# Attention on one core: q and k split as one 128-row tile, their copies made in two rounds, and heads stored in pairs

## The reference

```python
scores = q @ k.T / sqrt(64)                     # q, k, v: (4, 8, 576, 64) float32
thresh = scores.max(-1) - tau
attn = exp(where(scores >= thresh, scores, -1e9) - scores.max(-1))
attn = attn / (attn.sum(-1) + 1e-9)
x = (attn @ v) -> rows (4 * 576, 8 * 64)        # then the two expert layers
```

## Time and profile before

| what | value |
|---|---|
| median of three runs | 1363.23 us (1362.61 to 1364.46) |
| the profiled execution, its own time | 1361.96 us |
| its span, first to last instruction | 1359.8 us |
| attention | from 0 to about 385 us of the span |
| one iteration of the loop (four heads) | about 45 us |
| q1 queue (SP), share of 16 DMA engines' span | 20.2% |
| DMA share between 205 and 250 us | 0.41, 97 GB/s |

### The profile page before, as it was taken

One profiled execution on the slowest core, in us unless ns is written; L12 is line 12 of the kernel. 1 busy time (PEld: TensorE's weight loads), 2 busy tenths in 40 slices (PEclk: granted clock), 3 DMA queues, 4 the chain that ended last, 5 costly groups with the idle time before them and its releaser, 6 DMA issues.

```text
span 1359.8 us, 22119 instructions
## 1 busy us (share of the span) xinstructions
PE 1276.0 (94%) x7777; PEld 1147.4 (84%) x7777; DVE 652.3 (48%) x1256; ACT 560.0 (41%) x987; POOL 521.3 (38%) x372
## 2 busy tenths in 40 slices
PE   5999999999984799999999999994999999999998
PEld 4999999999842789989999998993999899899897
DVE  7999999999815211212121121114455445545443
ACT  3888888888842232333323333331221112112111
POOL 1777777777831252443434334344341101000000
PEclk9999999999987799999999999996999999999999
DMA  5443434343330332423324233233221102000000
GB/s 119 90 97 96 99 94 100 89 105 89 95 97 0 101 126 92 155 100 119 125 103 143 90 128 129 103 117 124 72 83 55 47 1 70 16 0 23 15 1 24
DMA packets 117483, 113.31 MB, mean 83 GB/s; under 512 B 74736, under 2 KB 84528, under 8 KB 117424
## 3 DMA queue, kind: packets, MB, share of 16 engines
q1 hardware_dynamic: 103552, 77.37, 20.2%
q0 software_dynamic: 6080, 19.93, 4.5%
q10 hardware_dynamic: 7792, 15.21, 3.1%
HBM read 81.90 MB, written 19.92 MB: 75 GB/s over the span
## 4 chain that ended last, share of the span: by engine, by line
PE 80%; DVE 8%; issue 4%; ACT 2%; POOL 2%; DMA 1%; SPq 1%; DVEq 0%; POOLq 0%; ACTq 0%
PE h_ps L629 31%; PE y_ps L647 10%; PE y_ps L646 10%; PE y_ps L648 10%; PE o_acc L516 4%; PE ring L477 3%; PE ring L490 3%; PE ring L478 2%; PE ring L491 2%; DVE k_parts L907 2%; PE t_ps L607 2%; ACT probs L711 1%; DVE neg_max L877 1%; PE logits_t_ps L558 1%; DVE q_lo L905 1%
## 5 line engine op out<-in xcount | busy, mean ns | idle before, releaser
L629 PE MATMUL h_ps<-x_hi,region_a 128*128 128x384 f32 (+1 forms) x1408 | 341.9, 315 | 2.8 <-DVE x_lo L1021 2.8
L1115 POOL TENSOR_TENSOR probs_lo<-probs,probs_hi 128x576 fp32r<-128x576 f32 x160 | 226.2, 1422 | 89.3 <-ACT probs_hi L719 89.1
L629 PEld LDWEIGHTS h_ps<-x_hi,region_a 128*128 128x128 f32 x1408 | 246.0, 189 | 9.2 <-DVE x_lo L1021 3.6
L629 PE MATMUL h_ps<-x_lo,region_a 128*128 128x384 f32 (+1 forms) x704 | 220.3, 313 | 0.0
L1031 DVE SCALAR_TENSOR_TENSOR h_lo<-h_ps,h_hi 128x256 fp32r<-128x256 f32 (+1 forms) x128 | 62.8, 491 | 318.7 <-ACT h_hi L805 318.7
L808 ACT ACTIVATE h_hi<-act_out 128x384 fp32r<-128x384 f32 (+1 forms) x112 | 53.7, 479 | 316.0 <-DVE act_out L1040 316.0
L647 PE MATMUL y_ps<-region_b,h_hi 128*128 128x512 f32 x448 | 176.3, 393 | 0.0
L648 PE MATMUL y_ps<-region_b,h_lo 128*128 128x512 f32 x448 | 176.0, 393 | 0.0
L646 PE MATMUL y_ps<-region_b,h_hi 128*128 128x512 f32 x448 | 175.7, 392 | 0.0
L1101 POOL TENSOR_TENSOR region_b<-stage,region_b 128x1024 fp32r<-128x1024 f32 x40 | 95.7, 2394 | 172.4 <-ACT region_b L700 172.3
L805 ACT ACTIVATE h_hi<-h_ps 128x256 fp32r<-128x256 f32 (+1 forms) x128 | 56.0, 438 | 243.4 <-PE h_ps L629 238.7
(11 more groups left out here) (161 smaller groups left out, 2438.8 us busy)
## 6 DMA issues: line engine op xcount, KB each, us to landing
stage<-in_moe_w SPq DMA_DIRECT2D x56, 512.0 KB, 3.5
expert_rows<-rows_out ACTq DMA_DIRECT2D x8, 768.0 KB, 3.8
q_hi<-q_hi SPq DMA_DIRECT2D x32, 160.0 KB
k_ones<-k_parts SPq DMA_DIRECT2D x32, 160.0 KB
qk_nat<-in_q SPq DMA_DIRECT2D x32, 128.0 KB, 2.7
qk_nat<-in_k SPq DMA_DIRECT2D x32, 128.0 KB, 2.7
v_nat<-in_v SPq DMA_DIRECT2D x16, 256.0 KB, 2.9
early<-in_moe_w SPq DMA_DIRECT2D x16, 256.0 KB, 3.1
```

Of the source, the lines that this page charges most:

```text
L629: mm = pe.matmul(h_ps[:, c % 2, 0:width], wt, x[kind][:, cc, :], start=(n == 0), stop=(n == 3 * C - 1))
L1115: pool.tensor_tensor(probs_lo[:, m % 4, :], probs[:, m % 4, :], probs_hi[:, m % 4, :].bitcast(F32), ALU.subtract).then_inc(lo_done, 1)
```

## The change

Instead of splitting q and k separately (two copies of 64 rows on ACT, two subtractions of 64 rows on DVE), ACT copies all 128 rows of the "qk" buffer into `q_hi2` = [q_hi; k_hi], and DVE subtracts all 128 rows into `k_parts` = [q_lo; k_lo] at once. Then a first round of two DMAs takes k_hi to `k_ones` and q_lo to `q_lo`; when both have landed (`parts_in`), a second round of two copies q_hi over k_hi in `q_hi2` and k_hi over q_lo in `k_parts`. The second round stands in slots c = 3 modulo 5 of SP's list. PE's S of the head waits for the second round. The row of zeros is no longer written for each head: the maxima stand two rows further down (rows D + 2 and D + 3), and two rows stay zero from the start, which makes the contraction 68 instead of 66 rows. The seven loads move from slots 0 and 10 to slots 1 and 11, behind the first round; `early` moves from slot 1 to slot 2. Two heads are stored together, in slots 4 and 14. `x_head` now lies in the memory of `stage`, which is used only after attention.

```diff
-        max_cols = sb("max_cols", [P, NT, D + 2], F32R)
+        max_cols = sb("max_cols", [P, NT, D + 4], F32R)
...
+        def copied_in(i, c):
+            return c // NT + 3 if c % NT == 3 else None
...  (SP)
                 if g is not None and has(i, g, NH, U):
                     s = g % U
-                    wait(sp, k_hi_done, head(i, g) + 1)
-                    sp.dma_start(q_lo[D:D + 2, s, :] ..., zero_rows[:, :] ...).then_inc(copies_in[g % 2], 16)
-                    sp.dma_start(q_hi2[D:P, s, :].bitcast(F32), q_hi2[0:D, s, :].bitcast(F32)).then_inc(copies_in[g % 2], 16)
-                    sp.dma_start(k_ones[0:D, s, :].bitcast(F32), k_parts[0:D, s, :].bitcast(F32)).then_inc(copies_in[g % 2], 16)
-                if c in (0, 2 * NT) and has(i, 0, NH, U) and has(i, U, NH, U):
-                    load_pair(i, U if c == 0 else U + 2)
+                    wait(sp, qk_hi_done, head(i, g) + 1)
+                    sp.dma_start(k_ones[0:D, s, :].bitcast(F32), q_hi2[D:P, s, :].bitcast(F32)).then_inc(parts_in[g % 2], 16)
+                    wait(sp, freed, past("qk", i, g))
+                    sp.dma_start(q_lo[0:D, s, :].bitcast(F32), k_parts[0:D, s, :].bitcast(F32)).then_inc(parts_in[g % 2], 16)
+                if c in (1, 2 * NT + 1) and has(i, 0, NH, U) and has(i, U, NH, U):
+                    load_pair(i, U if c == 1 else U + 2)
+                g = copied_in(i, c)
+                if g is not None and has(i, g, NH, U):
+                    s = g % U
+                    wait(sp, parts_in[s % 2], (head(i, g - s % 2) // 2 + 1) * 32)
+                    sp.dma_start(q_hi2[D:P, s, :].bitcast(F32), q_hi2[0:D, s, :].bitcast(F32)).then_inc(copies_in[s % 2], 16)
+                    sp.dma_start(k_parts[0:D, s, :].bitcast(F32), k_ones[0:D, s, :].bitcast(F32)).then_inc(copies_in[s % 2], 16)
...
-                if c == 1 and has(i, 0, NCH, 1):
+                if c == 2 and has(i, 0, NCH, 1):
                     wait(sp, first_w_lo, i * 2)
                     sp.dma_start(first_layer_part(early, i), ...).then_inc(first_w_in, 16)
                     sp.dma_start(second_layer_part(early, i), ...).then_inc(first_w_in, 16)
-                if j == 4 and has(i, c // NT - 1, NH, U):
+                if c in (NT - 1, 3 * NT - 1) and has(i, c // NT - 1, NH, U):
...  (both heads of the pair in one store, rows of 128 instead of 64 values)
...  (PE)
-                        wait(pe, copies_in[s % 2], (head(i, g - s % 2) // 2 + 1) * 48)
-                        wait(pe, freed, past("qk", i, g))
+                        wait(pe, copies_in[s % 2], (head(i, g - s % 2) // 2 + 1) * 32)
...  (ACT)
-                    act.activation(q_hi2[0:D, g % U, :], flat[0:D, 0:SP], ACT.Copy).then_inc(q_hi_done, 1)
-                    act.activation(k_parts[0:D, g % U, :], flat[D:P, 0:SP], ACT.Copy).then_inc(k_hi_done, 1)
+                    act.activation(q_hi2[:, g % U, :], ring[:, place("qk", i, g)].rearrange("p a n -> p (a n)")[:, 0:SP],
+                                   ACT.Copy).then_inc(qk_hi_done, 1)
...  (DVE)
-            dve.memset(zero_rows[:, :], 0.0)
-            dve.memset(max_cols[:, :, 0:D].bitcast(F32), 0.0)
+            dve.memset(q_lo[D:D + 4, :, :].bitcast(F32), 0.0)
+            dve.memset(max_cols[:, :, 0:D + 2].bitcast(F32), 0.0)
-            dve.memset(k_ones[D:D + 2, :, :].bitcast(F32), 1.0)
+            dve.memset(k_ones[D:D + 4, :, :].bitcast(F32), 1.0)
...
-                    wait(dve, q_hi_done, head(i, g) + 1)
-                    dve.tensor_tensor(q_lo[0:D, s, :], flat[0:D, 0:SP], q_hi2[0:D, s, :].bitcast(F32), ALU.subtract)
-                    wait(dve, k_hi_done, head(i, g) + 1)
-                    dve.tensor_tensor(k_parts[D:P, s, :], flat[D:P, 0:SP], k_parts[0:D, s, :].bitcast(F32),
-                                      ALU.subtract).then_inc(freed, 1)
+                    wait(dve, qk_hi_done, head(i, g) + 1)
+                    dve.tensor_tensor(k_parts[:, s, :], ring[:, place("qk", i, g)].rearrange("p a n -> p (a n)")[:, 0:SP],
+                                      q_hi2[:, s, :].bitcast(F32), ALU.subtract).then_inc(freed, 1)
```

More of the change, by code:

```diff
@@ L92, in build @@
         rden = sb("rden", [P, NT])
-        x_head = sb("x_head", [P, 2, NT, D])
+        x_head = stage[:, :, :].rearrange("p r n -> p (r n)")[:, 0:4 * NT * D].rearrange("p (b t g d) -> p b t g d", b=2, t=NT, g=2)
         ring = ps("ring", [P, 3, 2, 512])
@@ L101, in build @@
         v_in = [sem(f"v_in{i}") for i in range(2)]
-        qk_turned = sem("qk_turned"); q_hi_done = sem("q_hi_done"); k_hi_done = sem("k_hi_done")
+        qk_turned = sem("qk_turned"); qk_hi_done = sem("qk_hi_done")
+        parts_in = [sem(f"parts_in{i}") for i in range(2)]
         copies_in = [sem(f"copies_in{i}") for i in range(2)]
@@ L413, in slot_and_rows @@
                     if isinstance(i, int) and tile(i, c) == n:
-                        for s in x_out:
-                            sp.wait_ge(s, 16 * heads)
+                        for n, s in enumerate(x_out):
+                            sp.wait_ge(s, 32 * ((heads // 2 + 1 - n) // 2))
                         sp.wait_ge(first_w_lo, 2 * NCH)
@@ L422, in _ @@
             for s in x_out:
[L423 removed]
+                sp.wait_ge(s, 8 * NH)
             sp.dma_start(x_early[:, WHOLE:TOK, DM - 2 * D:DM], xr[:, WHOLE:TOK, DM - 2 * D:DM]).then_inc(x_in[2], 16)
@@ L490, in slot @@
                         pe.matmul(dst, k_parts[:, s, cols], q_hi2[:, s, half], start=True, stop=False)
-                        mm = pe.matmul(dst, k_ones[0:D + 2, s, cols], q_lo[0:D + 2, s, half], start=False, stop=True)
+                        mm = pe.matmul(dst, k_ones[0:D + 4, s, cols], q_lo[0:D + 4, s, half], start=False, stop=True)
                     mm.then_inc(st_ready, 1)
@@ L525, in slot @@
                     for t in range(FULL):
[L526 to L527 removed]
+                        mm = pe.matmul(at[0:D + 4, 1, t * P:t * P + P], max_cols[:, t, :], ident_r[:, :], start=True, stop=True)
+                    mm = pe.matmul(at[0:D + 4, 0, MAX_TAIL:MAX_TAIL + TAIL], max_cols[:, FULL, :], ident_r[:, 0:TAIL], start=True, stop=True)
                     mm.then_inc(max_turned, 1)
@@ L754, in slot @@
                     wait(act, max_turned, head(i, f) + 1)
-                    act.activation(q_lo[D:D + 2, f % U, 0:FULL * P], ring[D:D + 2, place("om", i, f), 1, :], ACT.Copy).then_inc(max_in, 1)
+                    act.activation(q_lo[D:D + 4, f % U, 0:FULL * P], ring[D:D + 4, place("om", i, f), 1, :], ACT.Copy).then_inc(max_in, 1)
             act.wait_ge(consts, 2)
@@ L913, in slot @@
                         wait(dve, o_turned, head(i, f - 2) + 1)
-                    dve.tensor_copy(q_lo[D:D + 2, f % U, FULL * P:S],
-                                    ring[D:D + 2, place("om", i, f), 0, MAX_TAIL:MAX_TAIL + TAIL]).then_inc(max_tail_in, 1)
+                    dve.tensor_copy(q_lo[D:D + 4, f % U, FULL * P:S],
+                                    ring[D:D + 4, place("om", i, f), 0, MAX_TAIL:MAX_TAIL + TAIL]).then_inc(max_tail_in, 1)
                     wait(dve, max_in, head(i, f) + 1)
@@ L921, in slot @@
                     wait(dve, o_turned, head(i, h) + 1)
-                    wait(dve, x_out[h % 2], head(i, h - h % 2) // 2 * 32)
+                    buf, side = h % U // 2, h % 2
+                    wait(dve, x_out[buf], head(i, h - h % U) // U * 32)
                     o = ring[:, place("om", i, f), 0, 0:NT * (D + 2)].rearrange("p (t n) -> p t n", t=NT)
```

32 lines of the change are left out of this document (14 added, 18 removed).

## The result

The changed kernel takes 1379.32 us (median of 4 runs, 1377.17 to 1380.72), the kernel before, run beside it again, 1362.92 us (1361.28 to 1364.46). The ratio is 1.0119, 95% interval 1.0099 to 1.0139. Forecast were 1360.4 us and a range of 1349 to 1371: the forecast was wrong, in sign and in range.

The account below looks back on a forecast made before the run. It took PE, busy 94% of the span, as the bound, with DVE near its limit in attention. Terms -22.6 + 15.8 + 0.7 + 3.3 = -2.8 us took 1363.23 to 1360.4 us, range 1349 to 1371.

Parts of the forecast that it names:

- the second step, "`early` comes later, and ACT is in order": Slot 5: ACT stands still for the late `early`, PE behind it; 2.25 us in seven iterations, 15.8 us lost.
- The split: Attention heads: one 128-row subtraction of 0.83 us ends PE's wait for DVE; 0.78 us in 29 heads, 22.6 us gained.
- ACT and `early`: ACT's wait in slot 5: last piece issued at 216.6, landed 2.9 us later, 2.25 us late; 15.8 us in all.
- rival B: Attention: `early` and copies both land later in a fuller shared queue; net +8 us, 1371.2 us; chance 0.24.
- The second round: Copies of slot 3, issued behind `early`: 1.4 us late for S, but hidden inside ACT's stall, so not charged.
- The copies of slot 13: Second-round copies behind seven loads: 0.1 us late for S, 0.7 us in seven iterations (bounds 0 and 5).
- Both stalls together: Attention: ACT's wait for `early`, 15.8 us, and the late copies of slot 13, 0.7 us.
- Start-up: Before attention: writing zeros into `q_lo` and the longer copies delay PE's first S by 2.6 us; 3.3 us in all.
- The sum on record: Whole kernel: -22.6 + 15.8 + 0.7 + 3.3 = -2.8 us, with no clock term.
- rival A: Attention: the stall for `early` does not bite, SP less late or the ring absorbs it; -18.6 us, 1344.6 us; chance 0.17.

Follow-up runs that it names:

- experiment 4: Changed kernel with 18 matmuls that nobody reads put into slot 7, ahead of PE's wait for the second round of copies: 1368.41 us, ratio 1.0043.
- experiment 2: Changed kernel with the seven loads back in slots 0 and 10, ahead of the first round of copies: 1345.65 us, ratio 0.9867.
- experiment 1: Changed kernel with the two loads of `early` moved ahead of the seven loads, in slot 1: 1358.27 us, ratio 0.9964.
- experiment 5: Kernel with the seven loads back in slots 0 and 10, with `early` issued in slot 4, behind the stores: 1382.79 us, ratio 1.0141.

## Why the prediction was wrong

**What failed is the second step, "`early` comes later, and ACT is in order", in its price for the stall.** It named the place, the order of SP, the transfer and the chain to PE, and all of that is in the profile. Then it priced the stall as PE's idle time alone: "with PE at its limit nothing is made up later". True, and not enough. PE works slower after it has stood still. The missing term is the granted clock, 16.5 us in the profiled execution (11 to 17.5 by the three accounts of experiment 4). In the profile before the clock reads 1.00 in every iteration of attention, and no wait of PE there (100 to 342 us) is longer than 0.3 us. But its start-up shows the effect. PE is idle ahead of its first S, and then a matmul of 288 columns starts every 0.24 us until about 20.4:

```profile
14.94 0.61 PE L477 MATMUL ring<-k_parts,q_hi 128*128 128x288 f32 x1 [5.02 <-DMA k_ones<-k_parts]
15.35 0.44 PE L478 MATMUL ring<-k_ones,q_lo 66*128 66x288 f32 x1
15.59 0.44 PE L477 MATMUL ring<-k_parts,q_hi 128*128 128x288 f32 x1
```

The clock column reads 1.00 in that stretch, so only the spacing tells. It was a reason to give the clock a range, and none was given. The other terms:

- *The split.* Right in kind and in duration. The groups by line, 0 to 400 us, for the changed kernel:

```profile
L912 DVE TENSOR_TENSOR k_parts<-ring,q_hi 128x640 fp32r<-128x640 f32 x32 | 26.1, 816 | 2.8 <-ACT q_hi L736 2.7
...
L736 ACT ACTIVATE q_hi<-ring 128x640 fp32r<-128x640 f32 x32 | 22.5, 704 | 21.1 <-PE ring L509 21.1
```

  0.816 us for 128 rows against a predicted 0.83 and 0.806 and 0.828 on 64; the copy has not changed. Gained are 18.1 us in 28 heads (experiment 2), 0.65 each, between the bounds of 0.55 and 0.81; I had said 0.78 (21.8 in 28). A head without a stall takes 10.4 to 10.8 us, where I wrote 10.4 to 10.6. A small new wait stands in place of the old one: in experiment 2 PE's weight load waits for GpSimd's `probs_lo` (5.1 us in 11, 100 to 342 us).
- *ACT and `early`.* ACT waits 24.2 us in seven, 3.46 each, and not 15.8. SP was priced well: its last issue for `early` begins 6.7 us behind the subtraction's end (231.82 against 224.34 + 0.82 = 225.16), and I had 6.7 too (216.6 against 209.9). The landing was not: 4.2 us passed until ACT could start (236.03 - 231.82), where I took 2.9 from an emptier queue. Over the eight iterations this piece lands 3.4 to 4.7 us after its issue (median 4.1); in the trace of before it was 3.0 to 4.8 (median 3.0), so a longer landing could be read there. That is the mechanism of rival B.
- *The second round.* I set it 1.4 us late and inside ACT's stall. PE in fact waits for it directly (2.36 us): it is issued at 232.94, and PE has nothing else to do from 234.6 on. In the chain of waits of the changed kernel:

```profile
232.94 3.88 DMA k_parts<-k_ones
```

  3.88 us from issue to landing behind `early`, 2.67 alone and 2.64 behind the loads in experiment 1. As the prediction took from the Trainium skill ("DMA: Bandwidth & Descriptors", section "Queues, rings and completion order"), each DMA engine consumes the descriptors of a queue in ring order; the later landing behind `early` agrees with it, and the row of the empty queue, which I preferred, was too low by 1.2 us. The copies of slot 13, for which the sum had 0.7 us in seven iterations, are late in the first one only: PE waits 1.75 us (69.72), and that head takes 12.6 us. In the other six iterations the same head takes 10.4 to 10.6 us.
- *Both stalls together*: 19.5 us at most by experiment 4 (1.9 of them at the one place of slot 17) against 16.5 in the sum (15.8 + 0.7). The idle time was therefore near the forecast, though ACT waits 24.2 us and not 15.8: its waits and PE's overlap.
- *Start-up.* PE's first S starts at 18.27, not 14.94: 3.3 us, where the sum had 3.3 and the text 2.6 for this place (17.5). The timelines of DVE, then PE:

```profile
2.08 2.19 DVE L865 MEMSET q_lo<- 4x2560 f32 x1 [0.57 <-issue]
```

```profile
9.34 2.36 PE L509 MATMUL ring<-ident,qk_nat 128*128 128x128 f32 x10 [9.34 <-DVE threshold L875]
18.27 0.61 PE L486 MATMUL ring<-k_parts,q_hi 128*128 128x288 f32 x1 [6.57 <-DMA k_parts<-k_ones]
```

  At the fourth head 2.1 us of it are left.

The account, for the profiled executions: -18.1 (gain) + 19.5 (stalls) + 16.5 (clock) + 2.1 (start) = +20.0 at the last head's subtraction, 364.74 against 344.77. The sum on record, taken to the same place (28 heads), was -21.8 + 16.5 + 3.3 = -2.0 with no term for the clock. Of the 22.0 us between, 3.7 are the smaller gain, 3.0 the longer stalls and 16.5 the clock; the start gives 1.2 back. Without the clock the change would have come out about 5 us slower, as experiment 4 does (1368.41 us, 1.0043, some of the fill perhaps in it): inside the range, but still not on the side of the forecast. Rival B saw the direction, a later landing of both, and priced it at 1371.2; it too lacked the clock. That rival A (1344.6, SP not late) meets experiment 2's 1345.65 is partly luck: its gain was too large by 3.7 us in 28 heads (21.8 against 18.1), and its start too dear by 1.6 (3.3 against 31.83 - 30.10 = 1.7).

## What to carry to other kernels

Where the engine at its limit is TensorE, price a new stall of 2 to 4 us, as these were, twice: once as idle time, and once more for the matmuls that follow at 1.2 GHz; give that second price a range from nothing to the same amount, since it didn't always come here. When loads are moved behind something in an in-order DMA queue, ask of each entry behind them which engine wants it and when, and take its landing time from a row in a full queue. A stall whose end can't be moved can be made cheaper by giving PE anything to do in it (10.9 us here).

## What the runs showed of the hardware

- **The granted clock after a stall.** PE idle for 2.4 us: then some 6.6 us with a matmul of 288 columns every 0.24 us instead of 0.133. In the changed kernel PE was idle for 2.0 to 2.9 us at seven places, and slow behind each, for a longer or a shorter time; behind the 1.75 us of 69.72 it was not. In experiment 1, behind 2.12 us, it worked from 67.72 to about 69.1 at full speed and only then slowly. The Trainium skill ("TensorE: Matmul & The Clock Gate", Part 1, "What's actually happening") has the low clock as the resting state that activity lifts. Experiment 4 agrees, where the same wait filled with unread matmuls leaves the clock at 1.00. The length of the idle time alone does not decide: 3.15 us in experiment 5 did not lower the clock:

```profile
232.43 0.30 PE L487 MATMUL ring<-k_ones,q_lo 66*128 66x288 f32 x1
235.88 0.40 PE L499 MATMUL ring<-q_hi,k_parts 128*128 128x288 f32 x1 [3.15 <-DVE probs L901]
236.11 0.30 PE L500 MATMUL ring<-q_lo,k_ones 68*128 68x288 f32 x1
236.25 0.30 PE L499 MATMUL ring<-q_hi,k_parts 128*128 128x288 f32 x1
```

- **Rows of these instructions cost nothing.** DVE's subtraction over 640 columns takes 0.816 us on 128 rows and 0.806 or 0.828 on 64; ACT's copy 704 ns and 698 or 704.
- **A queue's landing time is no constant.** The same copy of 160 KB lands 2.5 to 4.4 us after its issue in the changed kernel (median 2.7).
